# A hand-set order of a fused attention and MLP kernel: scaling behind exponentials, one unit's scores, one weight piece and nine products of zeros placed anew

## What is computed

```
def _attn_ref(q, k, v):
    q_d, k_d, v_d = (a.reshape(B, H, Sd, factor, D).mean(axis=3) for a in (q, k, v))
    out_up = np.repeat(sm_attn(q_d, k_d, v_d), factor, axis=2)
    mask = np.abs(pos[:, None] - pos[None, :]) < factor
    scores = np.where(mask, scale * np.matmul(q, k.transpose(0, 1, 3, 2)), -1e9)
    ...
    return out_up + out_local

h = np.maximum(np.maximum(x @ w1, x @ w2), x @ w3)     # x: 2304 x 512, w: 512 x 768
y = h @ w_out                                          # 768 x 512
h2 = y @ w_in; g = np.maximum(0.01 * h2, h2)           # 512 x 2048
out = g @ w_out2                                       # 2048 x 512
```

## Time and profile before

| | |
|---|---|
| median of 3 runs | 788.41 us (787.58 to 789.71) |
| the profiled execution | 790.14 us |
| its span in the trace | 788.4 us |
| mean granted clock of PE | 0.991 of full |
| PE busy | 768.7 us (98%) |
| PE weight loads busy | 689.7 us (87%) |
| DVE, ACT, POOL busy | 445.9, 296.2, 164.9 us |

### The profile page before, as it was taken

How to read it: one execution, slowest core, us unless ns; L and a number is a source line. 1 busy time by engine, 2 the same in 40 slices (tenths; PEclk the granted TensorE clock), 3 DMA queues, 4 the chain that set the end, 5 groups by cost and what they waited for, 6 DMA issues and landing times.

```text
span 788.4 us, 13523 instructions
## 1 busy us (share of the span) xinstructions
PE 768.7 (98%) x5404; PEld 689.7 (87%) x5404; DVE 445.9 (57%) x769; ACT 296.2 (38%) x697; POOL 164.9 (21%) x208
## 2 busy tenths in 40 slices
PE   8788999999999999999999999999999999999998
PEld 7677898988888888999998888888998899889986
DVE  6665588856674373566855656664434366334333
ACT  4464454433333233343544344452222244222222
POOL 4575222111101152441243345110000000000000
PEclk9899999999999999999999999999999999999999
DMA  8451343323212011422267455446243226322312
GB/s 293 131 211 38 94 135 101 119 74 102 66 47 76 1 54 54 123 62 81 89 235 304 174 190 232 165 160 228 94 145 136 94 93 216 145 95 94 143 44 81
DMA packets 37630, 98.91 MB, mean 125 GB/s; under 512 B 2880, under 2 KB 23360, under 8 KB 34496
## 3 DMA queue, kind: packets, MB, share of 16 engines
q1 hardware_dynamic: 37568, 98.05, 35.7%
HBM read 73.92 MB, written 24.12 MB: 124 GB/s over the span
## 4 chain that ended last, share of the span: by engine, by line
PE 92%; DVE 4%; ACT 2%; issue 1%; POOL 0%; DVEq 0%; ACTq 0%
PE mlp_ps L1067 10%; PE mlp_ps L1069 9%; PE mlp_ps L1068 9%; PE mlp_ps L1219 7%; PE mlp_ps L1221 7%; PE mlp_ps L1220 7%; PE att_ps L1240 6%; PE att_ps L1242 6%; PE att_ps L1241 6%; PE mlp_ps L1242 3%; PE mlp_ps L1241 3%; PE mlp_ps L1240 3%; PE att_ps L1139 2%; PE att_ps L1141 2%; PE att_ps L1140 2%; PE att_ps L1056 2%
## 5 line engine op out<-in xcount | busy, mean ns | idle before, releaser
L1067 PE MATMUL mlp_ps<-x_hi,wa_lo 128*128 128x288 f32 (+1 forms) x288 | 103.7, 360 | 2.0 <-POOL wa_lo L865 1.8
L1069 PE MATMUL mlp_ps<-x_hi,wa_hi 128*128 128x288 f32 (+1 forms) x288 | 99.1, 344 | 0.0
L1068 PE MATMUL mlp_ps<-x_lo,wa_hi 128*128 128x288 f32 (+1 forms) x288 | 98.8, 343 | 0.0
L1507 ACT ACTIVATE h_last_a<-wa_raw 128x384 fp32r<-128x384 f32 x72 | 37.7, 524 | 105.9 <-DVE wa_raw L1840 104.7
L1067 PEld LDWEIGHTS mlp_ps<-x_hi,wa_lo 128*128 128x128 f32 x288 | 55.7, 194 | 8.2 <-issue 2.0
L1838 DVE TENSOR_TENSOR wa_raw<-mlp_ps,h_raw 128x384 f32<-128x384 f32 x24 | 13.4, 558 | 86.5 <-PE mlp_ps L1221 54.1
L1069 PEld LDWEIGHTS mlp_ps<-x_hi,wa_hi 128*128 128x128 f32 x288 | 55.6, 193 | 4.5
L1068 PEld LDWEIGHTS mlp_ps<-x_lo,wa_hi 128*128 128x128 f32 x288 | 55.9, 194 | 4.0
L1852 DVE TENSOR_TENSOR h_last_b<-wa_raw,h_last_a 128x384 fp32r<-128x384 f32 x72 | 45.0, 631 | 22.5 <-ACT h_last_a L1507 20.5
L855 POOL TENSOR_TENSOR v_rows<-v_rows 72x512 f32<-72x512 f32 x16 | 20.9, 1306 | 153.3 <-DMA v_rows<-in_v_sum 153.3
L1242 PE MATMUL att_ps<-wa_hi,h_last_a 128*128 128x512 f32 x132 | 52.3, 396 | 0.0
(11 more groups left out here) (215 smaller groups left out, 2050.9 us busy)
## 6 DMA issues: line engine op xcount, KB each, us to landing
u_even<-u_scratch SPq DMA_DIRECT2D x8, 1792.0 KB, 7.2
u_odd<-u_scratch SPq DMA_DIRECT2D x8, 1792.0 KB, 7.3
kq_in<-in_kq SPq DMA_DIRECT2D x14, 576.0 KB, 3.8
u_scratch<-u_even SPq DMA_DIRECT2D x4, 1792.0 KB, 8.7
u_scratch<-u_odd SPq DMA_DIRECT2D x4, 1792.0 KB, 8.8
v_rows<-in_v_sum SPq DMA_DIRECT2D x16, 288.0 KB
wa_raw<-in_w SPq DMA_DIRECT2D x6, 768.0 KB, 6.0
v_win<-in_v_band SPq DMA_DIRECT2D x12, 384.0 KB, 3.4
```

Source lines behind the costliest of these rows:

```text
L1067: nc.tensor.matmul(ps, wlo, xhi, start=(n == 0), stop=False)
L1068: nc.tensor.matmul(ps, whi, xlo, start=False, stop=False)
L1069: last = nc.tensor.matmul(ps, whi, xhi, start=False, stop=(n == len(pairs) - 1))
L1507: nc.scalar.activation(g_tile(0, quad, part), g_raw[part], ACT.Copy).then_inc(g_hi_ready, 1)
```

## The change

Only the list of the first phase changes:

- the products of zeros between V 1 and T 2 become 13 instead of 4;
- the second half of weight tile 1, `("W", 1, 1)`, moves from behind V 3 to behind N 3;
- `("Mk", 3, 0, 3)`, the first nine products of the fourth group (group 3), moves behind S 4 and E 4;
- N of units 5, 6 and 7 goes from places 6.4, 10.2 and 13.9 to 7.0, 10.6 and 14.4, behind E of units 6, 7 and 8 (6.9, 10.5, 14.3).

```diff
--- before.py
+++ after.py
@@ -153,11 +153,11 @@
         ("Z", 8), ("D", 0), ("S", 0), ("Z", 5), ("E", 0), ("D", 1), ("D", 2), ("G", 0), ("S", 1), ("Z", 6), ("E", 1),
         ("LR", 2), ("G", 1), ("N", 0), ("S", 2), ("Z", 2), ("T", 0), ("Z", 3), ("W", 0, 0), ("E", 2), ("D", 3), ("LR", 3),
         ("G", 2), ("WL", 1), ("W", 0, 1), ("N", 1), ("V", 0), ("LV", 2), ("X", 0, 0), ("S", 3), ("Z", 2), ("T", 1),
-        ("Z", 3), ("E", 3), ("G", 3), ("W", 1, 0), ("N", 2), ("V", 1), ("Z", 4), ("LV", 3), ("WL", 2), ("T", 2), ("XH", 0, 1), ("N", 3),
-        ("XL", 0, 1), ("Mk", 0, 0, 1), ("Mk", 1, 0, 1), ("Mk", 2, 0, 1), ("V", 2), ("T", 3), ("D", 4),
+        ("Z", 3), ("E", 3), ("G", 3), ("W", 1, 0), ("N", 2), ("V", 1), ("Z", 13), ("LV", 3), ("WL", 2), ("T", 2), ("XH", 0, 1), ("N", 3),
+        ("W", 1, 1), ("XL", 0, 1), ("Mk", 0, 0, 1), ("Mk", 1, 0, 1), ("Mk", 2, 0, 1), ("V", 2), ("T", 3), ("D", 4),
         ("Mk", 0, 1, 2), ("Mk", 1, 1, 2), ("Mk", 2, 1, 2), ("LV", 4), ("WL", 3), ("X", 0, 2),
-        ("V", 3), ("W", 1, 1), ("D", 5), ("LV", 5), ("WL", 4), ("WL", 5), ("Mk", 0, 2, 3), ("Mk", 1, 2, 3), ("Mk", 2, 2, 3), ("Mk", 3, 0, 3),
-        ("X", 0, 3), ("S", 4), ("E", 4))
+        ("V", 3), ("D", 5), ("LV", 5), ("WL", 4), ("WL", 5), ("Mk", 0, 2, 3), ("Mk", 1, 2, 3), ("Mk", 2, 2, 3),
+        ("X", 0, 3), ("S", 4), ("E", 4), ("Mk", 3, 0, 3))
     for i in range(NF1):
         put(4, ("WL", NF1 + i))
     for c, at in ((2, 0.5), (3, 2.4), (4, 5.4), (5, 8.4)):
@@ -170,7 +170,7 @@
     put(1.5, ("LQ", 5))
 
 
-    plan = {4: (3.1, 5.4, 6.4, 7.7), 5: (6.4, 9, 10, 11.6), 6: (10.2, 12.8, 13.8, 15.6), 7: (13.9, 16.4, 20.1, 18.3),
+    plan = {4: (3.1, 5.4, 6.4, 7.7), 5: (7.0, 9, 10, 11.6), 6: (10.6, 12.8, 13.8, 15.6), 7: (14.4, 16.4, 20.1, 18.3),
             8: (18.5, 21.2, 22.4, 24.2), 9: (22.6, 25.2, 26.2, 28.2), 10: (26.2, 29.5, 30.5, 32.5), 11: (31.2, 34.5, 35.5, 37.5),
             12: (36.5, 40, 41.6, 43.7), 13: (43, 45.8, 46.7, 48.4), 14: (47.6, 50.3, 51.2, 52.9), 15: (52.1, 54.8, 55.7, 57.4),
             16: (57.5, 59.3, 62, 63.8), 17: (62.6, 65.6, 66.5, 68.3), 18: (67.4, 70.1, None, 72.4), 19: (71.9, 74.6, None, 76.4)}
```

## The result

The changed kernel takes 775.57 us (median of 4 runs, 773.53 to 778.43) where the kernel before, on the same chip, takes 788.00 (4 runs, 786.53 to 789.71). The ratio is 0.984, with a 95% interval from 0.981 to 0.988: 12.4 us faster. The forecast was 774.5, in a range from 771.5 to 780.5. The profiled execution of after took 774.59 us for a span of 772.8, and the one of before 790.14 for 788.4, so the two traces differ by 15.6 us where the medians differ by 12.4. That difference between the two differences is the subject of half of the experiments.

A forecast was written before the change was run, and what follows sets the result against it. TensorE has no slack from 85.3 us, so gains ahead of it reach the end one for one. 6.2 - 0.2 + 6.55 + 3.4 - 0.3 = 15.65 us off the profiled 790.1 gave 774.5, range 771.5 to 780.5.

The forecast's parts named there:

- the term for the zeros: Before unit 2's transposes: zeros fill PE's idle 2.09 us, keeping full clock from 27.3 to 34.1; gain 3.25 us.
- Rival (b): The clock falls all the same, zeros not counting as work or new idle falling badly: 777.8 or 779.5 us; chance 0.10.
- The path through T4: Unit 4's scores start at 34.1, its transposes at 42.6 after 0.6 us wait; the first part gives 6.2 us.
- The piece and the order: Ahead of unit 4's transposes: W(1,1) earlier removes PE's POOL wait, 1.76 us; scores before group 3's products, 1.35 less 0.1.
- The collision of x_lo and POOL: DVE's subtraction for unit 2 meets POOL's low part: costs 0.2 us, bounds 0 and 0.63.
- The waits of V4, V5 and V6: PE's waits for exponentials in the values of units 4, 5, 6 go: 2.06 + 2.23 + 2.26 = 6.55 us.
- Rival (c): PE's waits in the values of units 4 to 6 stay, something else ending them: 784.5 us; chance 0.05.
- The clock: Two half-clock stretches, at 68.2 and 81.9, return half their 3.4 us each: 3.4 us in all, bounds 0 and 3.4.
- T7's new wait: The second half of unit 7's transposes waits for unit 6's combination: costs 0.3 us, bounds 0 and 1.
- Rival (a): New PE waits at combinations, unit 4's transposes or POOL's low parts take part of the gain: 777.5 us; chance 0.10.
- Rival (d): Slower: many short PE waits keep the clock low through the first 70 us: 794.5 us; chance 0.03.

The follow-up runs named there:

- before_again: The kernel before, unedited, profiled in another execution: 786.49 us.
- m_zeros: The changed kernel with the products of zeros before unit 2's transposes back at 4 from 13: 775.73 us, ratio to before 0.984.
- m_scaling: The changed kernel with the scaling of units 5, 6, 7 back ahead of the exponentials of units 6, 7, 8: 784.18 us, ratio to before 0.996.
- more_pieces_g: more_pieces with POOL's value sums of unit 3 put behind the low part of weight piece W(1,0): 778.25 us, ratio to before 0.987.
- p_scaling: The kernel before with only the scaling of units 5, 6, 7 moved behind the exponentials of units 6, 7, 8: 778.42 us, ratio 0.989.
- p_piece_scores: The kernel before with only W(1,1) moved behind N 3 and group 3's first products behind S 4 and E 4: 784.17 us, ratio 0.996.
- p_zeros: The kernel before with only the products of zeros before unit 2's transposes at 13 in place of 4: 787.48 us, ratio 1.001.
- more_pieces: The changed kernel with four more ScalarE weight pieces moved (two of tile 0, one each of tiles 2 and 3): 773.78 us, ratio to before 0.982.
- after_again: The changed kernel, unedited, run again: 774.38 us, ratio to before 0.983.
- m_scores: The changed kernel with the first nine products of group 3 back ahead of the scores of unit 4: 777.35 us, ratio to before 0.987.

## Where the prediction was right and where it was wrong

**The total was right**, at 1.1 us above the forecast, though the term for the zeros was not. The four parts undone one at a time and made alone (medians and, for those alone, the ratio; then the counts from the traces, against after and `before_again`):

| part | undone in after | alone in before | in the traces | in the sum |
|---|---|---|---|---|
| zeros | +0.2 | +0.9 (ratio +0.5) | undone -0.1 | 3.25 |
| piece | +0.3 | with scores -2.4 (ratio -2.8) | undone +0.9; with scores -3.05 | 1.76 |
| scores | +1.8 | see piece | undone +1.05 | 1.35, less 0.1 |
| scaling | +8.6 | -8.1 (ratio -8.8) | undone +9.5, alone -9.6 | 6.55 + 3.4 - 0.3 |

**The zeros: the term of 3.25 us failed.** The prediction took the idle 2.09 us and the low stretch behind it as a property of the kernel. They came in one execution, with one of DVE's turns lost; 12 of 14 profiles lack it. Even there the 6.8 us at half clock cost less than 3.25: from S3 to T4 the first trace takes 3.68 us more than `before_again`, of which 0.95 is idle time before T2, so 2.7 for the clock. That the zeros "fill the stretch behind which the clock fell" holds, and that they cost nothing while ACT's N2 isn't ready; but N2 is ready about 0.9 us sooner as a rule, so the 26 records overrun it a little (T2 at 26.68 where N2 had ended by 25.9), without harm to T4 (23.93 us behind S3, 23.87 with 4 zeros). Rival (b) took this term out as well, but for another reason (zeros that don't count as work), and its 777.8 did not come. The forecast survived since it was made against the profiled execution, which was 1.7 us above the median, and kept as the end state rather than as a difference: 15.65 was forecast between the traces and 15.6 came. Between the medians 12.4 came. That 3.25 lacks there, just this term's size, is partly chance: the usual execution of before does have low stretches, only elsewhere and shorter ones, and the scaling's part measured 8.1 to 8.8 where its terms make 9.65 (9.6 between two traces).

**The path through T4 was right to 0.1 us, part of it by luck.** S4 at 34.07 (34.1 forecast), POOL's low parts of the third feature at 38.05 (38.1), T4 at 42.52 (42.6) after a wait of 0.77 (0.6). But S3 started 0.43 us later in after than in before, so counted from S3 the path was 0.5 us shorter than forecast (23.93 for 24.4). The piece and the order, 1.76 and 1.25, make 3.0, and 3.05 were measured. The split holds for one sequence only: with the scores in the old order the piece is worth 1.95 (26.93 - 24.98) and the scores then 1.05; with the scores moved first they are worth 2.1 (26.93 - 24.87) and the piece then 0.9. (The traces with 24.98 and 24.87 also have the zeros and the scaling, which by `m_zeros` and `m_scaling` don't move this count.) Both release the same chain.

**The collision of x_lo and POOL, 0.2 us, measured 0,** and its upper bound does not hold in every order. The row of DVE in after, beside a busy POOL (30.36 to 32.82):

```profile
31.90 0.46 DVE L1680 TENSOR_TENSOR x_lo<-x_raw,x_hi 128x288 fp32r<-128x288 f32 x1
```

That is the length with POOL idle. But `more_pieces_g` has 3.17 us for the same instruction. The bound of one POOL instruction, 0.63, took one POOL instruction for the most that DVE can lose. Nor do show what POOL did beside the 0.66 us: it ran L858, which ended at 21.74, and x_lo ended at 22.05.

**The waits of V4, V5 and V6, 6.55 us, were right**: they are gone in after and in `p_scaling`, and back in `m_scaling` with 2.06, 2.24 and 2.26 us. Rival (c) is out by this.

**The clock, 3.4 us for two stretches, was right in kind and too large.** The runs of before differ mostly by their clock. Over the 51 runs of before that stand beside the experiments, those with a mean clock of 0.995 to 0.997 (18 runs) average 786.2 us, those with 0.987 to 0.991 (20 runs) 789.7. A straight line through all 51 has 6.0 us for 0.01 of mean clock (standard error 0.6) and meets full clock at 783.4 us, which is an estimate, since no run of before had it. After has 774.5 at full clock (the mean of seven runs). By that line 8.9 us of the 12.4 are there at equal clock, and 3.5 are clock: before's median loses 4.6 to it, and after's 1.1. The sum's terms without the clock make 1.76 + 1.25 - 0.2 + 6.55 - 0.3 = 9.06, and its clock terms 3.25 + 3.4 = 6.65. So it is the clock that was mis-sized. A stretch of 3.4 us at half clock takes 1.7 / 788 = 0.0022 off the mean clock, and so costs 1.3 us by the line, not the 1.7 of the prediction. Pairs of traces say the same: 1.44 (`p_piece_scores` against `m_scaling`), 1.40 (`p_zeros` with one stretch between S3 and T4, against `before_again` with none), and 0 in `p_scaling`, where T4's wait took it up. Why the others cost less than half wasn't tested.

**T7's new wait, 0.3 us, was about 0.1.** Its second half (68.83) starts 0.4 behind the first (68.43), where the halves of T4 lie 0.3 apart. The range was right too, though its lower end, 771.5, doesn't follow from what it names: 772.8 without the 0.6 us of T4's wait is 772.2. Rival (a) did not come: T5 and M6 have no idle time before them. Rival (d) did not come. What came nearest to it is `more_pieces_g`, where moving POOL's sums made one wait of 2.31 us, with 6.8 us at half clock, and lost 4.5 us to `more_pieces`; it is one long wait, not many short ones.

## What to carry to other kernels

Behind an engine that is always busy, look for instructions that wait for a third engine and stand in a queue in front of work that is ready; putting them one place back gave two thirds of this change. Before a term of a sum is built on an idle stretch or a low clock, see whether a second execution of the same kernel has it: here 3.25 us of 15.65 were built on one instruction that lost its turn in one run. What a move is worth depends on which moves are already made when they release the same chain: the piece is worth 1.95 us ahead of the scores' move and 0.9 behind it. And where runs scatter more than the effect, count between two fixed points of the traces.

## What the runs showed of the hardware

**One DVE instruction beside POOL has several lengths.** The subtraction for x_lo takes 0.45 us alone. Beside a busy POOL it took 0.46 (after, at 31.90), 0.64 to 0.66 for the first of the four parts in ten profiles (0.88 in one, 1.12 to 1.13 in three), and 3.17 in `more_pieces_g`. DVE and POOL of `more_pieces` show one more:

```profile
31.67 1.32 DVE L1680 TENSOR_TENSOR x_lo<-x_raw,x_hi 128x288 fp32r<-128x288 f32 x1
```
```profile
27.66 5.02 POOL L865 TENSOR_TENSOR wa_lo<-wa_raw,wa_hi 128x192 fp32r<-128x192 f32 x8
```

It ends at 32.99, 0.31 behind POOL's end at 32.68, as the one of 3.17 us ends 0.32 behind. The 0.66 us of the earlier trace rows end 0.31 behind POOL's L858, and the 1.12 us of `more_pieces` (from 21.43) 0.31 behind L855, which ran from 20.98 to 22.24. In these four the subtraction ends 0.3 us behind the end of something that POOL did. That can be POOL's whole chain and not one of its instructions alone: in the 3.17 us POOL went through five. The Trainium skill ("SBUF — State Buffer", Who interferes with whom) has it that the loser is fully blocked for the whole instruction of the other and that issue order decides who blocks. The 1.24 us of L1643 beside the 1.28 of L855 agree with it, and so do the 0.78 us of L1633 in `after_again`, which started 0.53 us behind L855 and ended 0.04 behind it. The 3.17 us go beyond it. And in the ten profiles with the two side by side L1633 starts 0.02 to 0.03 us ahead of L855, both where it took 0.17 (23.09 and 23.12) and where it took 1.32 (24.09 and 24.11), so the recorded starts don't tell who wins. What decides between the lengths stays open.

**An idle stretch doesn't always bring the same clock.** The 2.06 us before V4 were followed by half clock in `m_scaling` and not in before, and about 1.55 before T4 in `before_again` (1.56) and not in before (1.53); an idle stretch of 2.74 us before S3 in the profile of `after_again` was followed by none. In `m_scores`, whose trace has no wait over 1.55 us, half the runs had a lower mean clock, and in after two of four had 0.997 and 0.998.
